# mLSTM attention, soft MoE and a SoLU layer on one core: the first stage in float32 row and column halves, with q and k transposed ahead

## The chip, the cores and the metric

One core of one Trainium2 chip. The time is the device time of one launch in microseconds (us); lower is better. The numbers are the median of three runs and one profiled execution. Engines are named as in the profile: PE (TensorE), PEld (its weight loads), DVE (VectorE), ACT (ScalarE), POOL (GpSimd), SP (SyncE, which issues the DMAs).

## The reference

B = 4 batches, H = 8 heads, S = 768 tokens, head size D = 40, so DM = H x D = 320. Three parts follow one another; the change is in the first.

```python
for t in range(S):                                   # mLSTM, per batch and head
    m_new = max(f_gate[t] + m, i_gate[t])
    f_stab, i_stab = exp(f_gate[t] + m - m_new), exp(i_gate[t] - m_new)
    C = f_stab * C + i_stab * outer(v[t], k[t])
    n = f_stab * n + i_stab * k[t]
    y[t] = sigmoid(o_gate[t]) * (C @ q[t]) / max(abs(n @ q[t]), 1)
x = y.reshape(3072, 320)
logits = x @ phi                                     # soft MoE: 8 experts of 4 slots
d, c = softmax(logits, axis=0), softmax(logits, axis=1)
x = c @ experts(d.T @ x)                             # relu(s @ w1[e]) @ w2[e]
h = x @ w_in                                         # SoLU layer, width 1024
out = layernorm(h * softmax(h), no_mean_shift) * g_ln @ w_out
```

## The kernel before

**Work and tiles.** The tokens are cut into NC = 6 chunks of L = 128. One tile is a chunk of one batch with its 8 heads; the NT = 24 tiles run chunk by chunk, and in a chunk over the B = 4 batches. Inside a tile the recurrence is a matrix product: P = (K Q^T) x W, where W[s, t] is the exponential of gate sums (causal), the numerator is P times values (with a column of ones for the denominator, so HV = 41 columns per head) plus the state of the earlier chunks times q, scaled by a coefficient. Then the state is decayed and k times the decayed values is added.

**Precision.** All matmuls of this stage run in bf16, and every float32 operand is split into a high and a low part. `high` and `low` (L246, L250) read the upper and the lower half of float32 words as bf16. q and k are split and packed to 128 columns per head: Q3 = (qh, qh, ql, 0) and K4 = (kh, kl, kh, kl). ACT writes the high parts (`q_high` L887, `k_high` L897), DVE the low ones (`q_low` L1046, `k_low` L1056). PE transposes both (L612, L613) and ACT copies the result to QKT (L920). So one matmul over 128 rows gives three of the four products of a score (L646), and the state, stacked as C3 by ACT and DVE (L948, L1142), takes q's three parts in one matmul (L654). P is split by DVE (`p_low`, L1075), v by POOL (L455), the decayed values by POOL (L477), x by POOL (L522) and phi once at the start. So P times values is four bf16 matmuls per head (L673 to L676), the update four per head (L690 to L693), x is transposed in six bf16 transposes (L707) and the logits are twelve matmuls (L720).

**Order of the work.** Each engine runs its own list of steps, written by hand: a unit is half a tile (4 heads, UNITS = 8 per chunk), and `step(c, k)` calls the functions of that engine in order, each on the unit that lies its lag behind (`live`, `half`, `tile_of`). The first chunk and the last are written out, the four between are a loop on each engine (`attention_steps`, L254), with addresses from registers. Engines wait for each other by semaphores (`wait_ge`, `then_inc`). DVE's step is at L1202: product of P (L1067), scaling of the state part (L1085), `sum_up` (L1097), low part of P (L1075), |n q| (L1106), q's low part, k's low part, maximum with one (L1115), addition to the state (L1133), reciprocal (L1124), stacked state (L1142). POOL's step decays values (L467) and state (L486), splits them, splits x, gates (L498), splits v and divides (L511). ACT takes the exponentials (L906) and the copies out of PSUM.

**DMAs.** SP loads each tile's q, k and v in one DMA of 484 KB (L337) and one w1 matrix (1280 KB) after each chunk (L363, L364). Behind the stage (`after_attention`) it loads the last two w1, w_out, w2[0] and w_in (L368 to L371), after si_done w2[1] to w2[3] (L374), and after w1_used w2[4] to w2[7] (L377). The expert products L790 (w1) and L822 (w2) are float32 matmuls in four column groups, and for the last 64 rows in two row halves; L802 and L774 are float32 transpositions by matmul with an identity. L822's second half waits for w2[4] to w2[7]. The last stage (from L854) is not touched.

## Time and profile before

| | |
|---|---|
| median of 3 runs | 377.07 us (376.53 to 378.76) |
| profiled execution, its time | 377.63 us |
| its span, first to last instruction | 375.9 us |
| mean granted TensorE clock | 0.909 of 2.4 GHz |
| busy share of the span | PE 74%, PEld 53%, DVE 83%, ACT 64%, POOL 69% |
| DMA | 56.61 MB, mean 151 GB/s |

The span is what the trace covers; the time of the execution is a little more, and the median is that of other runs. A busy share says how long an engine had an instruction in it, not that it set the pace; PE's ends are modelled.

### The profile page before, as it was taken

The page shows a single profiled execution, that of the slowest core. Times are in us where ns is not written, and L with a number is a line of the kernel's source. Part 1 is how long each engine was busy: PE and PEld are TensorE (multiplying, and loading weights), DVE is VectorE, ACT ScalarE, POOL GpSimd, SP SyncE. Part 2 cuts the span into 40 slices and gives each one's busy share as a digit, 9 for nine tenths or more (in the row PEclk, how much of TensorE's full clock was granted, in tenths as well). Part 3 has the DMA queues.
Part 4 walks back from the last instruction along what each step waited for, and adds up shares of the span by engine and source line. Part 5 has one row for each costly group of instructions (what it writes and reads, how often), then busy time and mean ns, then how long its engine had stood idle before and what let it go on. Part 6 is the DMA issues. An engine that isn't in the chain of part 4 may idle for free.

```text
span 375.9 us, 10868 instructions
## 1 busy us (share of the span) xinstructions
PE 279.9 (74%) x3881; PEld 200.6 (53%) x3881; DVE 312.7 (83%) x483; ACT 240.3 (64%) x402; POOL 259.6 (69%) x420
## 2 busy tenths in 40 slices
PE   0048687777878768787787449864838999999996
PEld 0036576666766657576675323421214666666664
DVE  8979999999999999999999654830179999999961
ACT  3857587866678577677766315350158989898970
POOL 4824999988898888889955500941028888888880
PEclk9999988989889698998989859986996999999999
DMA  7901115315113421512450079993009889899994
GB/s 291 365 0 54 56 55 196 107 55 190 55 53 98 157 95 53 192 53 58 138 246 3 2 282 413 418 424 142 0 4 152 175 189 194 181 175 183 201 187 131
DMA packets 62144, 56.61 MB, mean 151 GB/s; under 512 B 52320, under 2 KB 56416, under 8 KB 59552
## 3 DMA queue, kind: packets, MB, share of 16 engines
q1 hardware_dynamic: 62112, 56.19, 51.7%
q8 instruction: 19, 0.31, 0.4%
q14 instruction: 13, 0.11, 0.1%
HBM read 39.66 MB, written 3.93 MB: 116 GB/s over the span
## 4 chain that ended last, share of the span: by engine, by line
DVE 39%; PE 23%; issue 16%; POOL 9%; DMA 7%; ACT 3%; DVEq 1%; SPq 0%; POOLq 0%; ACTq 0%
DVE arena L1056 6%; DMA ring<-w_dram 6%; DVE arena L1142 4%; DVE arena L1106 4%; DVE arena L1115 4%; DVE arena L1067 3%; DVE arena L1075 3%; DVE arena L1097 3%; POOL ring L580 3%; POOL ring L574 3%; PE ps L822 2%; PE ps L863 2%; DVE arena L1133 2%; PE ps L864 2%; PE ps L690 2%
## 5 line engine op out<-in xcount | busy, mean ns | idle before, releaser
L863 PE MATMUL ps<-wouth,ring 128*128 128x320 bf16 x192 | 54.3, 306 | 1.6 <-DMA ring<-ring 1.4
L864 PE MATMUL ps<-woutl,ring 128*128 128x320 bf16 x192 | 54.2, 305 | 0.0
L920 ACT COPY arena<-ps 128x1024 bf16<-128x1024 bf16 x48 | 49.2, 1026 | 5.9 <-PE ps L613 5.6
L612 PE MATMUL ps<-identb,arena 128*128 128x128 bf16 x192 | 30.8, 240 | 24.4 <-DVE arena L1056 24.3
L906 ACT ACTIVATE arena<-ps 128x512 f32<-128x512 f32 x48 | 29.0, 605 | 15.9 <-PE ps L633 15.7
L1075 DVE TENSOR_TENSOR arena<-arena 128x512 bf16<-128x512 f32 x48 | 39.1, 814 | 0.0
L690 PE MATMUL ps<-arena 128*128 128x41 bf16 x160 | 19.2, 187 | 25.8 <-DVE arena L1133 25.8
L1067 DVE TENSOR_TENSOR arena<-ps,arena 128x512 f32<-128x512 f32 x48 | 32.0, 666 | 5.5 <-PE ps L646 3.3
L498 POOL TENSOR_TENSOR arena<-arena,sig 128x320 f32<-128x320 f32 x24 | 27.4, 1142 | 12.5 <-DVE arena L1097 12.3
L1305 DVE TENSOR_REDUCE ring<-ps 128x1 f32<-128x1024 f32 x24 | 29.3, 1223 | 6.1 <-PE ps L854 6.1
L1031 ACT ACTIVATE ring<-ring 128x1024 bf16<-128x1024 f32 x24 | 27.6, 1149 | 10.4 <-POOL ring L593 10.4
L612 PEld LDWEIGHTS ps<-identb,arena 128*128 128x128 bf16 x192 | 20.8, 109 | 24.6 <-issue 24.6
L673 PE MATMUL ps<-arena 128*128 128x41 bf16 x192 | 24.2, 186 | 11.1 <-DVE arena L1075 11.1
L1056 DVE TENSOR_TENSOR arena<-arena 128x640 bf16<-128x640 f32 x24 | 31.2, 1300 | 0.0
L613 PE MATMUL ps<-identb,arena 128*128 128x128 bf16 x192 | 30.7, 239 | 0.0
L690 PEld LDWEIGHTS ps<-arena 128*128 128x128 bf16 x160 | 15.9, 99 | 27.4 <-issue 22.9
L867 PE MATMUL ps<-wouth,ring 128*128 128x320 bf16 x192 | 30.0, 299 | 0.0
L1313 DVE SCALAR_TENSOR_TENSOR ring<-ps,ring 128x1024 f32<-128x1024 f32 x24 | 29.2, 1215 | 0.2
L571 POOL TENSOR_TENSOR ring<-ring 128x512 bf16<-128x512 f32 x24 | 28.3, 1179 | 0.9 <-ACT ring L1027 0.9
L467 POOL TENSOR_TENSOR arena<-arena 128x328 f32<-128x328 f32 x20 | 22.3, 1114 | 9.1 <-ACT arena L911 9.1
L1018 ACT ACTIVATE ring<-ps,ring 128x1024 f32<-128x1024 f32 x24 | 26.3, 1095 | 2.8 <-DVE ring L1305 2.8
L863 PEld LDWEIGHTS ps<-wouth,ring 128*128 128x128 bf16 x192 | 19.1, 100 | 15.8 <-DVE ring L1328 6.4
(206 smaller groups left out, 1126.5 us busy)
## 6 DMA issues: line engine op xcount, KB each, us to landing
ring<-w_dram SPq DMA_DIRECT2D x10, 1280.0 KB, 8.1
arena<-qkv_dram SPq DMA_DIRECT2D x24, 484.0 KB, 3.4
sig<-o_gate_dram SPq DMA_DIRECT2D x3, 1280.0 KB, 9.1
arena<-w_dram SPq DMA_DIRECT2D x3, 1280.0 KB, 8.1
sig<-w_dram SPq DMA_DIRECT2D x3, 1280.0 KB, 15.2
out_dram<-ring SPq DMA_DIRECT2D x24, 160.0 KB, 2.3
arena<-w_out_dram SPq DMA_DIRECT2D x1, 1280.0 KB, 12.6
arena<-w_in_dram SPq DMA_DIRECT2D x1, 1280.0 KB, 14.1
```

The costliest lines, as they stand in the source:

```text
L612: pe.transpose(dst[:, j, :], Q3[b][:, h * QW:h * QW + P], identb[:, :])
L613: last = pe.transpose(dst[:, HALF + j, :], K4[b][:, h * KW:h * KW + P], identb[:, :])
L690: pe.matmul(bX[:, cols], first, high(VD[b % 2][:, cols]), start=True, stop=False)
L863: pe.matmul(o, UHT[i % 4][:, j, :], wouth[:, j, :], start=(j == 0), stop=False)
L864: pe.matmul(o, UHT[i % 4][:, j, :], woutl[:, j, :], start=False, stop=False)
L867: mm = pe.matmul(o, ULT[i % 4][:, j, :], wouth[:, j, :], start=False, stop=(j == FJ - 1))
L920: act.copy(QKT[k % 2], bT[k % 2].bitcast(BF16)).then_inc(s["t_copied"], 1)
L1056: dve.tensor_tensor(k4[:, :, :, 1, :], again(heads(tin[b][:, DM:2 * DM], D), 2, 2), k4[:, :, :, 0, :], ALU.subtract).then_inc(s["k_lo"], 1)
L1067: dve.tensor_tensor(PF[(k - 1) % 2], bS, WT[(k - 1) % 2], ALU.mult).then_inc(s["p_ready"], 1)
L1075: dve.tensor_tensor(low(pf), pf, high(pf), ALU.subtract).then_inc(s["pl_ready"], 1)
L1305: dve.tensor_reduce(nmx[i % 3], h_banks(i), AX.X, ALU.max, negate=True).then_inc(s["mx_ready"], 1)
L1313: dve.scalar_tensor_tensor(out=UT[i % 3], in0=h_banks(i), scalar=1.0, in1=ET[i % 2], op0=ALU.mult, op1=ALU.mult, accum_out=usum[i % 3]).th ...
```

## The change

q and k now come from the host already transposed (`qkT`: for each tile two halves of 4 heads, 40 rows, q's and k's columns), and k and v with its ones by token (`kv1`). The split, packing, transposing and copying of q and k on ACT, DVE and PE go, and so do the stacked state C3, the split of the decayed values, of x and of phi. Scores, queries times state, the update, the transposes of x and the logits are float32 matmuls. Heads 0 to 3 lie on rows 0 to 39 and heads 4 to 7 on rows 64 to 103 of the array; PE takes them in turn (`for r in range(2)` inside `for j`), the scores of the two halves into two PSUM banks. The state is 104 rows by 164 columns, and its update writes its two halves from two column halves. P and v stay split in bf16. A step is a whole tile; all loops are written out. The denominator is one reduction over |n q| and a column of ones. The copy of the logits moves from ACT to DVE, the decay of the values reads W's last column instead of exponentials of its own. `num`, `den`, `rden8` and `scaled` have two buffers, W and P two whole tiles. SP loads a tile in three DMAs and a w1 matrix after every second tile, all eight ahead of `after_attention` (the last two went behind it before).

```diff
--- before.py
+++ after.py
...
-        def attention_steps(eng, step):
-            for k in range(UNITS):
-                step(0, k)
-            with eng.Fori(1, NC - 1) as c:
-                for k in range(UNITS):
-                    step(c, k)
-            for k in range(UNITS):
-                step(NC - 1, k)
-            for k in range(UNITS - 1):
-                step(NC, k)
-
...
+        FLUSH = 5
+
+        def attention_steps(step):
+            for n in range(NT + FLUSH):
+                step(n)
...
+            def load_tile(i):
+                b = i % B
+                for r in range(2):
+                    sp.dma_start(qk[b][r * UPPER:r * UPPER + D, :], qkT[i, r]).then_inc(qk_in[b], 16)
+                sp.dma_start(kv[b], kv1[i]).then_inc(kv_in[b], 16)
...
+            for i in range(B, NT):
+                sp.wait_ge(s["i_done"], i - B + 1)
+                sp.wait_ge(s["o_done"], i - B + 1)
+                sp.wait_ge(s["x_done"], i - B + 1)
+                load_tile(i)
+                if i % 2:
+                    e = (i - B) // 2
+                    if e < RING:
+                        sp.dma_start(ring[:, e, :], w1[e]).then_inc(s["w1_first_in"], 16)
+                    elif e < E:
+                        sp.dma_start(w1_place(e), w1[e]).then_inc(s["w1_late_in"], 16)
 
             after_attention(sp)
-            for e in range(RING, E):
...
+            def decay_values(n):
...
+                pool.wait_ge(s["w_ready"], 2 * i + 2)
                 await_(pool, "x_done", i - 1)
-                vd = VD[b % 2]
-                pool.tensor_tensor(heads(vd, HV), heads(v1, HV), again(kdec[b % 2], 2, HV), ALU.mult) \
+                last_token = heads(WT[i % 2], L)[:, :, L - 1]
+                pool.tensor_tensor(heads(VD[i % 2], HV), heads(values_of(b), HV), again(last_token, 2, HV), ALU.mult) \
                     .then_inc(s["vd_ready"], 1)
...
-            def step(c, k):
-                decay(c, k)
-                decay_state(c, k)
-                decayed_low(c, k)
-                x_low(c, k)
-                gate(c, k)
-                split_v(c, k)
-                divide(c, k)
...
+            def step(n):
+                decay_values(n)
+                decay_state(n)
+                split_v(n)
+                gate(n)
+                divide(n)
...
-                await_(pe, "t_copied", n - 1)
-                dst = bT[parity(k)].bitcast(BF16).rearrange("p (j t) -> p j t", t=P)
+            def exponents(n, hf):
+
+                i = tile_at(n, 0)
+                if i is None:
+                    return
+                c, b = i // B, i % B
+                head = b * H + HALF * hf
+                await_(pe, "w_ready", 2 * i + hf)
+                pe.matmul(bE, identb[:, :], causal[:, :], start=True, stop=False)
+                pe.matmul(bE, A3[0:G3, c * L:(c + 1) * L], pick[:, head:head + HALF, :], start=False, stop=False)
                 for j in range(HALF):
-                    h = HALF * hf + j
-                    pe.transpose(dst[:, j, :], Q3[b][:, h * QW:h * QW + P], identb[:, :])
-                    last = pe.transpose(dst[:, HALF + j, :], K4[b][:, h * KW:h * KW + P], identb[:, :])
-                last.then_inc(s["t_done"], 1)
...
+            def scores(n):
...
+                pe.wait_ge(qk_in[b], 32 * (i // B + 1))
+                await_(pe, "p_ready", 2 * i)
                 for j in range(HALF):
-                    last = pe.matmul(bS[:, j * L:(j + 1) * L], qkt[:, HALF + j, :], qkt[:, j, :],
-                                     start=True, stop=True)
+                    for r in range(2):
+                        last = pe.matmul(bS[r][:, j * L:(j + 1) * L], keys_of(b, r, j), queries_of(b, r, j),
+                                         start=True, stop=True)
                 last.then_inc(s["s_done"], 1)
-                if hf == 0:
-                    await_(pe, "i_scaled", i)
-                await_(pe, "c3_ready", i - B + 1)
+                await_(pe, "i_scaled", i)
+                await_(pe, "state_ready", i - B + 1)
                 for j in range(HALF):
-                    h = HALF * hf + j
-                    last = pe.matmul(bI[:, h * HV:(h + 1) * HV], qkt[:, j, :], C3[b][:, h * HV:(h + 1) * HV],
-                                     start=True, stop=True)
+                    for r in range(2):
+                        last = pe.matmul(bI[r][:, j * HV:(j + 1) * HV], queries_of(b, r, j),
+                                         state[b][r * UPPER:r * UPPER + D, j * HV:(j + 1) * HV],
+                                         start=True, stop=True)
                 last.then_inc(s["i_done"], 1)
 
...
-            def add_to_state(c, k):
...
+            def logits(n):
...
+                for kk in range(NP):
+                    last = pe.matmul(bX[:, 400:400 + SLOTS], XT[i % 2][:, kk, :], phif[:, kk, :],
+                                     start=(kk == 0), stop=(kk == NP - 1))
+                last.then_inc(s["lg_done"], 1)
...
+            def add_to_state(n):
...
+                pe.wait_ge(s["vd_ready"], i + 1)
                 await_(pe, "state_ready", i)
-                for h in range(H):
-                    cols = slice(h * HV, (h + 1) * HV)
-                    first, second = K4[b][:, h * KW:h * KW + P], K4[b][:, h * KW + D:h * KW + D + P]
-                    pe.matmul(bX[:, cols], first, high(VD[b % 2][:, cols]), start=True, stop=False)
-                    pe.matmul(bX[:, cols], first, low(VD[b % 2][:, cols]), start=False, stop=False)
-                    pe.matmul(bX[:, cols], second, high(VD[b % 2][:, cols]), start=False, stop=False)
-                    last = pe.matmul(bX[:, cols], second, low(VD[b % 2][:, cols]), start=False, stop=True)
+                await_(pe, "lg_ready", n - 4)
+                pe.wait_ge(s["coefs_ready"], 3)
+                for j in range(HALF):
+                    for r in range(2):
+                        h = r * HALF + j
+                        last = pe.matmul(bX[r * UPPER:r * UPPER + D, j * HV:(j + 1) * HV], kv[b][:, h * D:(h + 1) * D],
+                                         VD[i % 2][:, h * HV:(h + 1) * HV], start=True, stop=True)
                 last.then_inc(s["x_done"], 1)
 
...
+            def transpose_x(n):
...
+                for kk, r0 in enumerate(PARTS):
+                    last = pe.transpose(bM[:, kk * P:(kk + 1) * P], sig[:, i, r0:r0 + P], identf[:, :])
                 last.then_inc(s["xt_done"], 1)
...
-            def step(c, k):
-                exponents(c, k)
-                transpose_qk(c, k)
-                scores(c, k)
-                if isinstance(c, int) and (c, k) == (0, 1):
+            def step(n):
+                exponents(n, 0)
+                scores(n)
+                exponents(n, 1)
+                if n == 0:
                     coefficients()
-                weigh_values(c, k)
-                add_to_state(c, k)
-                transpose_x(c, k)
-                logits(c, k)
+                weigh_values(n)
+                logits(n)
+                add_to_state(n)
+                transpose_x(n)
...
+            def denominator(n):
                 dve.wait_ge(s["num_ready"], i + 1)
-                nq = heads(num, HV)[:, :, D]
-                dve.scalar_tensor_tensor(out=den, in0=nq, scalar=-1.0, in1=nq, op0=ALU.mult, op1=ALU.max) \
-                    .then_inc(s["abs_ready"], 1)
...
+            def copy_logits(n):
+                dve.wait_ge(s["lg_done"], i + 1)
+                dve.wait_ge(s["x_done"], min(n, NT - B))
+                dve.tensor_copy(lg[:, i, :], bX[:, 400:400 + SLOTS]).then_inc(s["lg_ready"], 1)
...
-            def step(c, k):
-                p_product(c, k)
-                if isinstance(c, int) and (c, k) == (0, 2):
+                for r in range(2):
+                    rows = slice(r * UPPER, (r + 1) * UPPER)
+                    last = dve.tensor_copy(gamma[rows], heads(bX[rows, 0:NT * H], H, NT)[:, :, r * HALF:(r + 1) * HALF])
+                last.then_inc(s["coefs_ready"], 1)
+                dve.wait_ge(s["coefs_ready"], 2)
+                dve.memset(bX, 0.0).then_inc(s["coefs_ready"], 1)
+
+            def step(n):
+                p_product(n, 0)
+                if n == 0:
                     copy_coefficients()
-                scale_inter(c, k)
-                sum_up(c, k)
-                p_low(c, k)
-                absolute(c, k)
-                q_low(c, k)
-                k_low(c, k)
-                at_least_one(c, k)
-                add_state(c, k)
-                invert(c, k)
-                stack_state(c, k)
...
```

PE in the first stage, before: two half-tile steps in the loop (L612, L613: transposes of q and k; L646 scores; L654 queries times state).

```order
L630 MATMUL ps<-causal,identb 128x512
L631 ISA
L631 MATMUL ps<-pick_words,arena 128x512
L633 ISA
L633 MATMUL ps<-arena,pick_words 128x128 x4
L612 MATMUL ps<-identb,arena 128x128
L613 MATMUL ps<-identb,arena 128x128
...
L643 REGISTER_ALU
L646 MATMUL ps<-arena 128x128 x4
L654 MATMUL ps<-arena 128x41 x4
```

PE in the first stage of the changed kernel, from the logits of one step into the next (L602 logits, L619 update, L631 transposes of x, L543 to L546 exponents, L560 scores, L567 queries times state).

```order
L602 MATMUL ps<-phif,arena 128x32 x3
L619 MATMUL ps<-arena 40x41 x8
L631 MATMUL ps<-identf,sig 128x128 x3
L543 MATMUL ps<-causal,identb 128x512
L544 MATMUL ps<-pick_words,arena 128x512
L546 MATMUL ps<-arena,pick_words 128x128 x4
L560 MATMUL ps<-arena 128x128 x8
L567 MATMUL ps<-arena 128x41 x8
L543 MATMUL ps<-causal,identb 128x512
L544 MATMUL ps<-pick_words,arena 128x512
L546 MATMUL ps<-arena,pick_words 128x128 x4
```

The transposes of q and k and the register instructions are gone, the scores of all 8 heads stand together between the two halves of the exponents, and logits, update and transposes are 3, 8 and 3 instructions.

DVE in the first stage, before: one tile is two half-tile steps of the loop (L1056 k's low part, L1142 stacked state, L1106 and L1115 the denominator, L1046 q's low part).

```order
L1067 TENSOR_TENSOR arena<-ps,arena 128x512
L1085 TENSOR_TENSOR arena<-ps,arena 128x328
L1075 TENSOR_TENSOR arena<-arena 128x512
L1056 TENSOR_TENSOR arena<-arena 128x16x40
L1142 SCALAR_TENSOR_TENSOR arena<-arena,lo_rows_c 128x328
...
L1097 TENSOR_TENSOR arena<-arena,ps 128x328
...
L1106 SCALAR_TENSOR_TENSOR arena<-arena 128x8
L1046 TENSOR_TENSOR arena<-arena 128x8x40
L1115 TENSOR_SCALAR arena<-arena 128x8
L1133 TENSOR_TENSOR arena<-arena,ps 128x328
L1124 RECIPROCAL arena<-arena 128x8
```

DVE in a step of the changed kernel (L896 product, L914 scaling, L904 low part, L924 sum, L933 denominator, L951 addition to the state, L960 copy of the logits).

```order
L896 TENSOR_TENSOR arena<-ps,arena 128x512
L914 TENSOR_TENSOR arena<-ps,arena 128x328
L904 TENSOR_TENSOR arena<-arena 128x512
L896 TENSOR_TENSOR arena<-ps,arena 128x512
L924 TENSOR_TENSOR arena<-arena,ps 128x8x41
L904 TENSOR_TENSOR arena<-arena 128x512
L933 TENSOR_REDUCE arena<-arena 128x8
L942 RECIPROCAL arena<-arena 128x8
L951 TENSOR_TENSOR arena<-arena,ps 104x164
L960 COPY lg<-ps 128x32
```

Of the thirteen instructions of a tile ten are left, one of them new here (L960), and the addition to the state has half the elements.

## Rows read from the trace of the kernel before

**Rows 1.** Windows: stretch, its us, busy us (records) by engine, clock, DMA, GB/s.
```profile
60.00:80.00 20.00, 15.86 (x313) 13.69 (x314) 20.00 (x34) 13.44 (x27) 17.96 (x22) 0.83 0.27 90
...
250.00:376.00 126.00, 107.77 (x754) 65.02 (x746) 86.39 (x124) 80.59 (x124) 78.30 (x193) 0.94 0.76 155
```

**Rows 2.** Timeline of DVE: start us, us, engine line op out<-in.
```profile
84.53 0.69 DVE L1067 TENSOR_TENSOR arena<-ps,arena 128x512 f32<-128x512 f32 x1 [0.20 <-issue]
...
92.60 0.63 DVE L1067 TENSOR_TENSOR arena<-ps,arena 128x512 f32<-128x512 f32 x1
```

**Rows 3.** Groups of DVE, 60 to 120 us: busy us, mean ns | idle before.
```profile
L1075 DVE TENSOR_TENSOR arena<-arena 128x512 bf16<-128x512 f32 x15 | 12.7, 847 | 0.0
L1056 DVE TENSOR_TENSOR arena<-arena 128x640 bf16<-128x640 f32 x8 | 10.8, 1344 | 0.0
L1067 DVE TENSOR_TENSOR arena<-ps,arena 128x512 f32<-128x512 f32 x15 | 10.0, 664 | 0.7 <-issue 0.6
L1142 DVE SCALAR_TENSOR_TENSOR arena<-arena,lo_rows_c 128x328 bf16<-128x328 bf16 x7 | 7.2, 1027 | 0.0
L1115 DVE TENSOR_SCALAR arena<-arena 128x8 f32<-128x8 f32 x8 | 5.6, 696 | 0.0
L1106 DVE SCALAR_TENSOR_TENSOR arena<-arena 128x8 f32<-128x8 f32 x7 | 5.4, 770 | 0.0
L1085 DVE TENSOR_TENSOR arena<-ps,arena 128x328 f32<-128x328 f32 x8 | 3.9, 484 | 0.0
```

**Rows 4.** Timeline of PE, first stage, from L690 to L612.
```profile
84.28 0.19 PE L690 MATMUL ps<-arena 128*128 128x41 bf16 x1 [0.74 <-DVE arena L1133]
...
85.41 0.38 PE L630 MATMUL ps<-causal,identb 128*128 128x512 bf16 x1
...
86.06 0.22 PE L612 MATMUL ps<-identb,arena 128*128 128x128 bf16 x1
```

**Rows 5.** Timeline of PE, and groups of PEld (217 to 262 us), behind the first stage.
```profile
237.28 0.60 PE L790 MATMUL ps<-ring,arena 128*8 128x512 f32 x2
...
237.82 0.60 PE L790 MATMUL ps<-ring,arena 64*8 64x512 f32 x2
...
237.86 0.60 PE L790 MATMUL ps<-arena 64*8 64x512 f32 x2
...
238.26 0.60 PE L790 MATMUL ps<-ring,arena 64*8 64x512 f32 x2
...
239.57 1.97 PE L802 MATMUL ps<-identf,pick_words 128*128 128x32 f32 x16 [0.68 <-ACT pick_words L999]
...
L802 PEld LDWEIGHTS ps<-identf,pick_words 128*128 128x128 f32 x16 | 1.9, 191 | 1.6 <-ACT pick_words L999 1.6
...
L774 PEld LDWEIGHTS ps<-sum,arena 128*64 128x64 f32 x4 | 0.2, 134 | 0.0
```

**Rows 6.** Groups of POOL, 60 to 120 us.
```profile
L486 POOL TENSOR_TENSOR arena<-arena 128x328 f32<-128x328 f32 x8 | 10.3, 1285 | 0.0
...
L455 POOL TENSOR_TENSOR arena<-arena 128x328 bf16<-128x328 f32 x8 | 8.5, 1061 | 0.0
...
L498 POOL TENSOR_TENSOR arena<-arena,sig 128x320 f32<-128x320 f32 x7 | 8.2, 1171 | 1.2 <-DVE arena L1097 1.1
...
L511 POOL TENSOR_TENSOR sig<-arena 128x320 f32 x8 | 5.8, 723 | 0.0
```

**Rows 7.** Groups of ACT, 60 to 120 us.
```profile
L906 ACT ACTIVATE arena<-ps 128x512 f32<-128x512 f32 x15 | 9.1, 605 | 5.2 <-PE ps L633 5.2
```

**Rows 8.** Chain that ended last, behind the first stage; timeline row of DVE L1187.
```profile
217.33 0.19 ACT lg L938
...
235.79 23.13 DMA ring<-w_dram
...
259.06 1.23 PE ps L822 x5
...
21.91 0.95 DVE L1187 TENSOR_TENSOR arena<-ring 32x768 bf16<-32x768 f32 x1
```

More of the change, by code:

```diff
@@ L432, in _ @@
             pool.wait_ge(s["im_ready"], 1)
-            for b in range(1, B):
-                pool.memset(C3[b], 0.0)
-            for b in range(B):
-                pool.memset(state[b], 0.0)
             pool.wait_ge(s["ll_ready"], 1)
```

582 lines of the change are left out of this document (202 added, 380 removed).

## The prediction

> **What bounds the kernel now.** The profiled execution takes 377.63 us, 1.7 more than its span of 375.9 and 0.6 more than the median of the runs shown; I reckon in the span and set the difference right at the end. A change of under about 1% (3.8 us) can't be told from none here.
>
> I read the busy time by windows first, since the change touches only the first stage. In a window of it DVE is busy 20.00 of 20.00 us, PE 15.86, POOL 17.96, ACT 13.44 [rows 1]: the first stage is bound by DVE. The DVE timeline gives its rate: the same place of the step, the first product of P in a tile, starts at 84.53 and at 92.60 [rows 2], so a tile takes 8.07 us, and 24 tiles fill the time up to the last copy of logits, which ends at 217.52 (217.33 + 0.19) [rows 8]. The groups of DVE say what a tile pays: two products (L1067) of 0.66, two low parts of P (L1075) of 0.85, k's low part (L1056) 1.34, the stacked state (L1142) 1.03, three of L1085's size at 0.48 and q's low part about the same, and two instructions on eight elements, L1106 and L1115, that take 0.77 and 0.70 [rows 3]. These sum to more than 8.07 because the end of one overlaps the start of the next. Last I read the chain behind the stage: 23.13 us of it is the landing of the last w2 loads, after which L822 starts at 259.06 [rows 8].
>
> **The change part by part.** *DVE.* L1056, q's low part, L1142, L1106 and L1115 go; one small reduction replaces the last two, and a copy of the logits comes over from ACT. What is left per tile: 2 x 0.66, 2 x 0.85, scaling and sum 2 x 0.48, adding to the state 0.24 to 0.48 (half the elements of 0.48), and three small ones, for which I take 0.2 each, the size of the logit copy [rows 3, 8]. Sum 4.8 (5.1 at most).
>
> *POOL.* v's low part 1.06, values times decay 1.1 (as L455), gate 1.17, division 0.72, decay of a state half as long 0.64 (half of L486; 1.29 if length doesn't count): 4.7, at most 5.3 [rows 6]. The low parts of x and of the decayed values, and the dummy instruction, go. *ACT.* Two exponentials of 0.61 [rows 7] and one copy: under 2 us. None of these three reaches what PE needs, next.
>
> *PE.* All bf16 work on q, k, state and logits becomes float32. The trace of before has float32 matmuls behind the stage, and there each is two passes (L802's 8 matmuls are 16 records [rows 5]). These sixteen passes with 128 columns of weights and 32 moving columns take 1.97 us, their weight loads 1.9 where one takes 0.191 [rows 5]: (1.9 - 0.19)/15 = 0.11 us from load to load. The loads, not the 32 columns, set that. Streaming 512 columns takes 0.44 per pass (237.82 to 238.26) [rows 5], so 128 columns take 0.11: a pass of the scores is 0.11 either way. Per tile, then:
> - exponents, twice, unchanged: 85.41 to 86.06, 0.65 each [rows 4]: 1.30.
> - scores: 8 matmuls, 16 passes of 0.11. If the two row halves run side by side 0.89, if one after another 1.78. Rows 5 speak for side by side: L790's 64-row matmuls have eight records (four rows of two) starting between 237.82 and 237.86, and the other eight 0.44 later. One row half (c2) has only four column groups in use, so eight at once means that the two row halves ran together. I take 0.89.
> - queries times state: 16 passes with 128-column loads, 0.89 or 1.78. Here loads weigh, not streams. L774, two column halves of 64, has four loads in 0.20 where one takes 0.134 [rows 5]; one after another, 0.055 apart, they would span 0.30. Loads of different parts of the array overlap. I take 0.89.
> - state update: 8 matmuls with 40 columns of weights in two column halves, like L774: 16 passes, 0.4 to 0.8, I take 0.5.
> - P times values: unchanged, 32 passes. With 12 passes of the logits they fill 84.28 to 85.41 [rows 4], 0.0257 each: 0.82.
> - logits: 6 passes of 0.11, 0.67 (12 of 0.026 before); transposes of x: 3 at 0.11, 0.33 (up to 0.64 if such a transposition streams like two passes).
> - changes between whole array and halves: L790 goes from 128-row to 64-row form between 237.28 and 237.82, 0.54, where a pass takes 0.44 [rows 5]: 0.1 each. There are four per step: 0.4.
>
> Sum 5.8 us at the full clock. The Trainium skill, TensorEngine Tiling (Array Packing), section Key Properties, says that a change of tiling mode drains TensorE. The trace agrees in that there is a gap, of 0.10; a drain of the 0.17 us that the skill's TensorE: Matmul & The Clock Gate gives as the fixed part of a single matmul would, as an estimate, make the step 0.3 and the kernel 6 us longer. It changes no term here.
>
> *Clock.* In the first stage of before the granted clock is 0.83 with PE busy 79%; in the last stage, with PE busy 86%, 0.94 [rows 1]. PE as the bound should look like the latter: 12% of the time at 1.2 GHz, where exponents, scores and P times values take nearly twice as long (about 8.3 us a step). 1/(0.88/5.8 + 0.12/8.3) = 6.0 us. I take 6.0 per tile; PE becomes the bound.
>
> *No ring of waits is longer.* Scores of tile n+1 wait for both products of tile n: from the start of scores n, 0.89 + 0.89 + 0.65 + exponential 0.61 + product 0.66 and four handovers, 3.9 of the 6.0. P times values n-1, logits n-4, update n-1 and transposes n-3 stand between and fill PE. The exponents wait for an exponential that ended 2 us earlier. Behind PE's wait for the update's decayed values (L434 of the changed POOL order) stand only the transposes, and the values are ready a step ahead.
>
> *Ends of the stage.* The rows are ready when L1187 ends, at 22.86 (21.91 + 0.95) [rows 8]; before, q's and k's low parts came next, now the first exponents start at once. The first step has no tile behind it and waits for coefficients, their copies and a memset: 2.4 us over a steady step (in the first step DVE adds four copies and the memset between its two products). After the last step has started: 3.3 for exponents, scores and exponents, 2.4 for exponential, product, sum and low part, 0.8 P times values, 0.5 sum, 1.2 gate, 0.7 division, 0.3 transposes, 0.5 copy, 0.7 logits, 0.2 copy, less what overlaps: 10.6. End: 22.9 + 2.4 + 23 x 6.0 + 10.6 = 173.9 against 217.5, so -43.6.
>
> *DMA.* A tile's load grows from 484 KB in one to about 644 KB in three, and a 1280 KB weight load follows every second one; at 0.38 MB/us (twelve loads of 1280 KB in 41.4 us behind the stage, see below) that is about 3.5 us of a 6 us step on average. A load is issued more than a step before its first reader: I cost it nothing; if it came 1 us late each time, 24 us. Two of twelve weight loads move out of the stretch behind the stage into cover. Twelve took from 217.5 to 258.9 (235.79 + 23.13) [rows 8], 3.45 each: -6.9, less about 0.7 for the queue's gap before si_done: -6.2. What is late next there is L822's first half, which would end near 250 on the old scale, before the new 252.8.
>
> Sum: 375.9 - 43.6 - 6.2 = 326.1 span, 327.8 as time of such an execution, 327 as median.
>
> **The rivals.** *A, partial overlap or waits between tiles*: scores run side by side, but the loads of queries times state take turns (+0.9), step 6.9: 23 x 0.9 = 21 us more, 348. For it: the loads' overlap is seen only on column halves. *B, POOL or DVE bound*: the gaps at changes of form vanish behind loads and the clock stays full; PE 5.3, POOL at 4.7 to 5.3: step 5.3, 311. *C, no change*: row halves take turns for everything: 1.30 + 1.78 + 1.78 + 0.82 + 0.67 + 0.8 + 0.33 + 0.4 = 7.9, 8.0 with clock, 44 + 4 us more than the forecast: 375. Against it the eight records at 237.82. *D, slower*: PE's clock. Weight loads of 0.11 against streams of 0.03 could leave the array counted as idle, and the clock at 1.2 GHz throughout: exponents 2.6, scores 1.7, state 0.9, P times values 1.1, logits 0.7, update 0.6, transposes 0.6, changes of form 0.8: 9.0, 23 x 3.0 and 4 at the ends more: 400. It decides from a step of 8.2 us on. Against it: two thirds of the step are streams or short bf16 passes.
>
> **How the numbers follow.** Forecast 0.55, A 0.20, B 0.13, C 0.07, D (with a late tile load on top of A) 0.05. Faster by over 1%: 0.88; within 1%: 0.07; slower: 0.05. The range reaches into A and B, and holds T from 5.2 to 7.3: 309 to 358.
>
> **What would show it.** Right: PE busy over 90% in the first stage, DVE under 85%; 16 score passes within 1 us, record pairs on the two row halves starting together; 5.8 to 6.2 us from step to step; last logits near 174; L822's second half 6 us closer behind it; ACT under 35% busy. Wrong: score passes 0.11 apart one by one (C), PE idle ahead of scores or updates with POOL or DMA as releaser, a granted clock under 0.8 (D), PE idle with POOL at 100% (B).

## The result and the profile after

The changed kernel takes 331.05 us in the median of four runs (328.48 to 331.48), the kernel before, timed with it, 376.8. The ratio is 0.876, with a 95% interval of 0.871 to 0.882: faster by 12.4%. Forecast were 327.0 us and a range of 309 to 358. The profiled execution takes 331.48 us, its span is 329.3.

Windows of the changed kernel, columns as in [rows 1], which holds the first of these windows of before:

```profile
60.00:80.00 20.00, 19.84 (x339) 17.40 (x342) 19.41 (x37) 6.08 (x11) 11.76 (x18) 1.00 0.77 253
80.00:100.00 20.00, 19.84 (x363) 17.60 (x365) 19.09 (x35) 5.62 (x10) 11.61 (x18) 1.00 0.69 217
```

PE went from 15.86 to 19.84 of 20 us and its granted clock from 0.83 to 1.00. DVE is still at 19.1 to 19.4, so from this view alone nobody could say which of the two sets the pace. ACT fell from 13.44 to 5.6 to 6.1, POOL from 17.96 to 11.7.

The PE timeline of one steady step (in the place of [rows 4]; columns start us, us, engine line op; a matmul row with x16 holds 16 passes, and the merged rows of single bf16 matmuls between 80.32 and 81.14 are left out):

```profile
79.65 0.39 PE L543 MATMUL ps<-causal,identb 128*128 128x512 bf16 x1
...
81.14 0.83 PE L602 MATMUL ps<-phif,arena 128*128 128x32 f32 x6
...
81.90 0.51 PE L619 MATMUL ps<-arena 128*40 128x41 f32 x16
...
82.34 0.55 PE L631 MATMUL ps<-identf,sig 128*128 128x128 f32 x3
...
83.48 1.16 PE L560 MATMUL ps<-arena 40*128 40x128 f32 x16
...
84.47 0.99 PE L567 MATMUL ps<-arena 40*128 40x41 f32 x16
...
85.39 0.39 PE L543 MATMUL ps<-causal,identb 128*128 128x512 bf16 x1
```

From L543 to L543 it is 5.74 us, against 8.07 before [rows 2]. Read start to start, as the durations overlap: exponents 0.67, P times values 0.82, logits 0.76, update 0.44, transposes 0.39, exponents with the change of form 0.75, scores 0.99, queries times state 0.92. (The transposes' 0.39 is the distance from L630 to L543, 88.29 to 88.68, in the run without the low-low product; here the record of L543 is missing.) No row has an idle time in brackets: PE waits for nobody, and for no tile load either.

The start is slower. The scores of the first, second and fourth tile:

```profile
23.64 2.08 PE L560 MATMUL ps<-arena 40*128 40x128 f32 x16
...
33.36 2.08 PE L560 MATMUL ps<-arena 40*128 40x128 f32 x16 [1.72 <-DVE arena L896]
...
49.73 1.16 PE L560 MATMUL ps<-arena 40*128 40x128 f32 x16
```

Sixteen passes take 2.08 us instead of 1.16 in the first three tiles, which is the level of 1.2 GHz. (The record of the granted clock begins with its first change, here at 49.7 us; before that the passes tell the level.) PE was busy 24.3 us of the 27 from 23 to 50 us. The kernel before also began its stage at the half level, but only for 4 us: a 512-column matmul takes 0.63 us at 25.07 and 0.39, as in the steady step, from 29.00 on.

```profile
25.07 0.63 PE L630 MATMUL ps<-causal,identb 128*128 128x512 bf16 x1
...
29.00 0.39 PE L630 MATMUL ps<-causal,identb 128*128 128x512 bf16 x1
```

The end of the stage, PE's timeline and the last copy of logits on DVE:

```profile
172.88 0.88 PE L631 MATMUL ps<-identf,sig 128*128 128x128 f32 x3
174.37 1.46 PE L602 MATMUL ps<-phif,arena 128*128 128x32 f32 x6 [0.61 <-ACT arena L805]
```

```profile
175.87 0.19 DVE L960 COPY lg<-ps 128x32 f32<-128x32 f32 x1 [2.58 <-PE ps L602]
```

The last tiles go through transposes, ACT's copy and logits one after the other (the last pass of P times values starts at 168.31, and four logits follow it, at 168.46, 170.26, 172.06 and 174.37), and the clock is granted at half from 172.6 on. The stage ends at 176.06 (175.87 + 0.19), where it was 217.52 [rows 8].

Behind it, two rows of PE's timeline, the first instruction behind those that si_done stands for, and the start of the second half of the w2 product:

```profile
187.52 0.41 PE L679 MATMUL ps<-arena,onesf 128*128 128x32 f32 x2
...
213.17 1.50 PE L733 MATMUL ps<-ring,arena 128*8 128x320 f32 x12 [4.49 <-DMA ring<-w_dram]
```

L733 is the old L822; its second half still waits for the w2 loads, 37.1 us behind the stage's end, where it was 41.5 (217.52 to 259.06) [rows 8].

### The profile page after: what moved, and what is told of

The parts are those of the page before. It is cut to its first block and busy times, and to the rows that moved or that the text cites. A ratio compares the mean times of both kernels' runs of the same rounds, so it can differ in the third digit from the quotient of the medians.

```text
span 329.3 us, 8741 instructions
## 1 busy us (share of the span) xinstructions
PE 276.9 (84%) x3311; PEld 202.9 (62%) x3345; DVE 256.8 (78%) x419; ACT 144.4 (44%) x222; POOL 174.3 (53%) x334
## 5 line engine op out<-in xcount | busy, mean ns | idle before, releaser
L904 DVE TENSOR_TENSOR arena<-arena 128x512 bf16<-128x512 f32 x48 | 64.9, 1351 | 0.0
L896 DVE TENSOR_TENSOR arena<-ps,arena 128x512 f32<-128x512 f32 x48 | 32.9, 686 | 10.9 <-ACT arena L797 8.2
L434 POOL TENSOR_TENSOR arena<-arena 128x328 f32<-128x328 f32 x20 | 15.0, 751 | 45.9 <-ACT arena L797 45.9
L560 PE MATMUL ps<-arena 40*128 40x128 f32 x384 | 30.6, 304 | 1.7 <-DVE arena L896 1.7
L543 PE MATMUL ps<-causal,identb 128*128 128x512 bf16 x25 | 10.6, 424 | 22.3 <-DVE arena L1006 22.3
L805 ACT COPY arena<-ps 128x384 f32<-128x384 f32 x24 | 11.5, 478 | 40.6 <-PE ps L631 40.6
L774 PEld LDWEIGHTS ps<-wouth,ring 128*128 128x128 bf16 x192 | 19.1, 100 | 15.6 <-DVE ring L1148 6.4
L560 PEld LDWEIGHTS ps<-arena 40*128 40x128 f32 x384 | 25.8, 204 | 4.6 <-issue 2.5
L466 POOL TENSOR_TENSOR sig<-arena 128x320 f32<-128x320 f32 x24 | 17.3, 722 | 20.1 <-DVE arena L942 19.7
L456 POOL TENSOR_TENSOR arena<-arena,sig 128x320 f32<-128x320 f32 x24 | 20.8, 865 | 10.7 <-DVE arena L924 10.7
L567 PE MATMUL ps<-arena 40*128 40x41 f32 x384 | 26.1, 285 | 0.0
L567 PEld LDWEIGHTS ps<-arena 40*128 40x128 f32 x384 | 26.0, 206 | 0.0
L875 ACT CAST ring<-ring 128x1024 bf16<-128x1024 f32 x24 | 24.8, 1033 | 0.2 <-DVE ring L1133 0.2
```

Of the source, the lines that this page charges most:

```text
L560: last = pe.matmul(bS[r][:, j * L:(j + 1) * L], keys_of(b, r, j), queries_of(b, r, j), start=True, stop=True)
L567: last = pe.matmul(bI[r][:, j * HV:(j + 1) * HV], queries_of(b, r, j), state[b][r * UPPER:r * UPPER + D, j * HV:(j + 1) * HV], start=True, ...
L774: pe.matmul(o, UHT[i % 4][:, j, :], wouth[:, j, :], start=(j == 0), stop=False)
L896: dve.tensor_tensor(PF[i % 2][:, cols], bS[hf], WT[i % 2][:, cols], ALU.mult).then_inc(s["p_ready"], 1)
L904: dve.tensor_tensor(low(pf), pf, high(pf), ALU.subtract).then_inc(s["pl_ready"], 1)
```

## The experiments

The times are medians of four executions; the kernel before stood at 376.8 to 378.8 us beside them. The profiled execution also gives the stage's end, which is the better measure of an edit of the stage: what lies between it and the end of the span came out near 153 us in some executions and near 155.5 in others, with the same instructions (153.2 in the changed kernel, 155.1, 156.0 and 155.5 in three of the runs below), as the clock was granted at half for more or less of it (a mean of 0.93 in the changed kernel's 153.2 us, 0.87 in the 155.1 and the 156.0, 0.89 in the 155.5).

**1. Is the start's loss the clock?** Warm-up:

```diff
+            pe.wait_ge(s["ll_ready"], 1)
+            for _ in range(30):
+                pe.matmul(bM, identb[:, :], causal[:, :], start=True, stop=True)
             pe.wait_ge(s["rows_ready"], 1)
```

> Thirty 512-column bf16 matmuls into an unused PSUM bank before the first exponents, started when LL is ready (about 13.7 us), so that PE's clock is at 2.4 GHz when the stage begins. Theory (the steps S0 to S3 of the changed kernel were 9.7, 8.2 and 8.2 us apart because the clock was at 1.2 GHz until 49.7 us): steps 1 to 3 fall to 5.7 to 7, last logits 5 to 7 us earlier, time 324 to 326 against 331. Rival (the first steps are slow because they wait for coefficients, loads and copies): under 2 us gained, 329 to 331. A second rival: the idle stretches of the first steps bring the clock down again, then the time stays at 331 too, but the records show short passes in the first scores only.

Measured: 327.51 us (327.05 to 328.75), 3.5 less. The first tiles' scores on PE, and a window:

```profile
22.94 1.16 PE L560 MATMUL ps<-arena 40*128 40x128 f32 x16
...
30.11 1.26 PE L560 MATMUL ps<-arena 40*128 40x128 f32 x16 [2.35 <-DVE arena L899]
```

```profile
31.00:38.00 7.00, 7.00 (x88) 5.49 (x86) 4.83 (x6) 1.00 (x2) 2.62 (x4) 0.51 0.09 25
```

The first step falls from 9.7 to 7.2 us and the stage ends at 169.79, 6.3 earlier. The three steps from the first to the fourth scores take 19.4 us (22.94 to 42.34) where the changed kernel takes 26.1. There is more to gain: the second scores stand 2.35 us idle for DVE's second product, and from 31.0 us on the clock is at half again for 7 us. Part of the median's gain is given back behind the stage (155.1 for 153.2). The kernels without warm-up differ too: in runs 6 and 8 below the clock rose near 40 us instead of 49.7, and the stage of run 6 ended 3.0 us earlier (173.06) at the same 5.74 us a step. Beside that execution the warm-up is worth 3.3 us of stage, not 6.3.

**2. Do the row halves overlap, and is it the order of issue that makes them?** Scores and queries times state, with the half as the outer loop:

```diff
-                for j in range(HALF):
-                    for r in range(2):
+                for r in range(2):
+                    for j in range(HALF):
                         last = pe.matmul(bS[r][:, j * L:(j + 1) * L], keys_of(b, r, j), queries_of(b, r, j),
...
-                for j in range(HALF):
-                    for r in range(2):
+                for r in range(2):
+                    for j in range(HALF):
                         last = pe.matmul(bI[r][:, j * HV:(j + 1) * HV], queries_of(b, r, j),
```

> Scores and queries times state with the row half as the outer loop and the head as the inner one: same 8 + 8 matmuls, same cost each, but four in a row on one row half. Theory (the overlap of the two halves comes from alternating them): scores go from 0.99 to about 1.8 us, queries times state from 0.92 to 1.8, the step from 5.74 to 7.4, time 331 + 23 x 1.7 = 369. Rival (the engine reorders enough to overlap anyway, or the halves never overlapped and a pass costs less than thought): 331 to 334.

Measured: 432.8 us, and 414 to 448 over its four executions: even the fastest is slower than the kernel before. The windows:

```profile
50.00:60.00 10.00, 10.00 (x169) 8.98 (x167) 9.72 (x18) 2.44 (x5) 5.58 (x9) 1.00 0.76 256
80.00:100.00 20.00, 20.00 (x171) 16.98 (x169) 8.55 (x18) 3.31 (x6) 4.06 (x6) 0.50 0.40 132
```

PE is busy all the time in both, but from 64.8 to 293.5 us, the rest of the stage (which ends at 282.97) and 10.5 us behind it, the clock is granted at half, and a step takes 11.41 us. While it was still full, scores and queries times state took 2.60 us (49.47 to 52.07), against 0.99 + 0.92 = 1.91 in alternating order, and a step was at most 6.42 (55.20 to 61.62). So the order itself costs 0.7 us a step, some 16 us; the other 85 are the clock. Thirty-two passes fully one after the other would take about 3.6 (32 x 0.11, an estimate). In this order the halves still overlap in part, where one half's last passes meet the other half's first. The rows show it where scores on rows 64 to 103 (L560) run beside states on rows 0 to 39 (L567):

```profile
50.58 0.30 PE L567 MATMUL ps<-arena 40*128 40x41 f32 x1
50.68 0.27 PE L560 MATMUL ps<-arena 40*128 40x128 f32 x1
50.71 0.28 PE L567 MATMUL ps<-arena 40*128 40x41 f32 x1
```

**3 and 4. Each group alone.** The scores' loops swapped, then those of queries times state.

> The row halves of the scores alone are issued one after the other (four heads of rows 0 to 39, then four of rows 64 to 103); queries times state keep the alternating order. With both in turn the two groups took 2.60 us at the full clock (49.47 to 52.07) in place of 1.91, so some overlap was left. Theory, the loads hide behind the streams less here, because a 128-column stream is as long as its load: +0.4 to +0.7 us per step at the full clock, +10 to +17 us, 341 to 348. Theory on the clock: it fell in the run with both in turn because the order leaves the array half used; then this half of the edit brings part of that, 360 to 400. Rival: the clock falls only with both, and the time stays under 350.

> The row halves of queries times state alone are issued one after the other; the scores keep the alternating order. Theory, here weight loads set the pace and those of one half follow each other, so less is hidden: +0.3 to +0.9 us per step at the full clock, +7 to +20 us, 338 to 351. If the clock falls as it did with both in turn, 360 to 400; rival: it costs nothing (under 333), and the scores' order was the whole of it.

Measured: 346.4 us (single executions 341.0, 343.7, 349.1 and 349.4; the trace is of the first) and 342.7 (342.35 to 343.12), both inside their ranges. The PE timelines, first of the scores in turn, then of the states in turn:

```profile
91.47 1.37 PE L560 MATMUL ps<-arena 40*128 40x128 f32 x13
...
93.94 0.39 PE L543 MATMUL ps<-causal,identb 128*128 128x512 bf16 x1
```

```profile
91.17 1.16 PE L560 MATMUL ps<-arena 40*128 40x128 f32 x16
...
93.55 0.39 PE L543 MATMUL ps<-causal,identb 128*128 128x512 bf16 x1
```

The pair takes 2.47 and 2.38 us in place of 1.91, the steps are 6.28 and 6.20, and the clock stays full in the stage in both. The rival held: the clock falls only with both.

**5. Is it the clock, and can more work bring it back?** Both groups in turn as in 2, and the product with the causal mask issued three times per half:

```diff
+                for _ in range(2):
+                    pe.matmul(bE, identb[:, :], causal[:, :], start=True, stop=True)
                 pe.matmul(bE, identb[:, :], causal[:, :], start=True, stop=False)
```

> Both groups with their row halves in turn, as in the run of 432.8 us, and in each half of the exponents the 128x512 product with the causal mask issued three times instead of once (the first two are overwritten): 4 more streams of 0.22 us, 0.89 us more work per step. Theory, the loss of that run was the clock: too much of its step were passes in which only a row half of the array moves data; with 0.89 us of full streams more in each step the clock stays at 2.4 GHz, the step is 6.42 + 0.89 = 7.3 us, and the time is 331 + 24 x (7.3 - 5.74) = 368 us: more work, 60 us less time. Rival, the fall was chance or comes from the step's length or the idle of other engines: the clock falls again, the step is above 12 us, and the time over 440.

Measured: 369.5 us (367.5 to 369.8), 63 us less than in 2 with 0.89 us more work per step. Its window and one step:

```profile
80.00:100.00 20.00, 20.00 (x279) 16.48 (x278) 15.51 (x28) 4.67 (x9) 8.61 (x13) 1.00 0.62 197
```

```profile
81.30 1.37 PE L562 MATMUL ps<-arena 40*128 40x128 f32 x13
...
83.90 0.61 PE L544 MATMUL ps<-causal,identb 128*128 128x512 bf16 x2
...
88.58 0.60 PE L562 MATMUL ps<-arena 40*128 40x128 f32 x3
```

Scores and states take the same 2.60 us (81.30 to 83.90), the step is 7.28, the clock full. So it was neither the length of that stretch nor that of the step; the full streams are all that was added, and they kept the clock up. What the chip measures there these runs don't say.

**6. Who sets the pace, PE or DVE?** First POOL kept away from DVE's second low part:

```diff
             def split_v(n):
...
                 b = i % B
+                if i > 0:
+                    pool.wait_ge(s["pl_ready"], 2 * i)
```

> POOL waits for both low parts of P of a tile before it splits v of the next. Theory (the second low part of P takes 2.26 us instead of 0.76 because it can't run beside POOL's row of four instructions; PE sets the pace, so it costs nothing): L904 falls to 0.76 us both times, DVE's busy share in the first stage from 95% to 70%, step still 5.74, time 330 to 332. Rival (DVE, busy 5.5 of 5.74 us, sets the pace as much as PE): the step falls by 0.1 or more, 325 to 329. A second rival for the mechanism (PE's reads of P slow DVE's write): L904 stays at 2.26.

Measured: 331.1 us (329.6 to 331.3), no change, and the step is 5.74 as before. DVE's and POOL's timelines in the changed kernel, and then DVE and POOL in this one:

```profile
80.19 0.76 DVE L904 TENSOR_TENSOR arena<-arena 128x512 bf16<-128x512 f32 x1
...
81.20 0.74 POOL L434 TENSOR_TENSOR arena<-arena 128x328 f32<-128x328 f32 x1 [1.36 <-ACT arena L797]
...
81.90 0.46 POOL L446 TENSOR_TENSOR arena<-arena 104x164 f32<-104x164 f32 x1
...
82.16 2.26 DVE L904 TENSOR_TENSOR arena<-arena 128x512 bf16<-128x512 f32 x1
82.32 0.73 POOL L423 TENSOR_TENSOR arena<-arena 128x328 bf16<-128x328 f32 x1
...
83.01 0.81 POOL L456 TENSOR_TENSOR arena<-arena,sig 128x320 f32<-128x320 f32 x1
```

```profile
84.05 0.80 DVE L906 TENSOR_TENSOR arena<-arena 128x512 bf16<-128x512 f32 x1
...
84.93 0.73 POOL L425 TENSOR_TENSOR arena<-arena 128x328 bf16<-128x328 f32 x1 [0.69 <-DVE arena L906]
```

The same instruction takes 0.76 us with POOL idle and 2.26 beside POOL's row L446, L423, L456, and ends at 84.42, 0.60 behind the row's end (83.82). With POOL behind it, it takes 0.80, and DVE's busy time falls from 19.1 to 14.6 of 20. So 1.5 us of DVE's 5.5 per step were a stall, not work; PE sets the pace.

**7. The same from PE's side.** The scores issued twice:

```diff
-                for j in range(HALF):
+                for j in [j for _ in range(2) for j in range(HALF)]:
```

> The 16 score passes of each tile are issued twice (same operands, same banks), nothing else is changed. Theory, PE sets the pace of the stage: the step grows by what the scores take there, 0.92 to 1.0 us, from 5.74 to 6.7, all 24 tiles of it: +22 to +24 us, about 354 us, with DVE's busy share in the stage falling from 19.2 of 20 to about 17. Rival, DVE (5.5 us of instructions per 5.74 us step) sets it as much as PE: PE has only 0.1 to 0.3 us to spare in that case too, so the step would be 6.4 or less and the time 346 or less. A second rival is the clock: with more passes of 40 rows in a step it could fall to 1.2 GHz inside the stage, as it did with the halves in turn; then over 365.

```profile
82.52 2.06 PE L560 MATMUL ps<-arena 40*128 40x128 f32 x32
...
89.15 1.05 PE L560 MATMUL ps<-arena 40*128 40x128 f32 x14
```

Measured: 354.6 us (351.2 to 358.8) for the 354 expected. The step is 6.63 (82.52 to 89.15): sixteen more passes cost 0.89, 0.056 each, half of the 0.11 of one whole-array pass. That is the overlap of the row halves, measured by itself.

**8. One matmul of four taken from P times values.** The product of the two low parts is left out, so the sum lacks that part:

```diff
                     pe.matmul(bO[:, cols], ph, vl, start=False, stop=False)
-                    pe.matmul(bO[:, cols], pl, vh, start=False, stop=False)
-                    last = pe.matmul(bO[:, cols], pl, vl, start=False, stop=True)
+                    last = pe.matmul(bO[:, cols], pl, vh, start=False, stop=True)
```

> P times values without the product of the two low parts: 24 bf16 passes of 41 columns per tile in place of 32 (the kernel leaves out that part of the sum). Theory, PE sets the pace: 8 x 0.0257 = 0.2 us less per step, 5.54, -4.9 us over the stage, about 326 us. DVE's instructions sum to 5.54 there, so DVE should be at 20 of 20 us busy and this is the last gain that PE alone can give. Rival, the step is held by DVE's second low part (2.26 us beside POOL's row): no gain, 330 to 331.

```profile
80.00:100.00 20.00, 20.00 (x344) 17.31 (x341) 19.88 (x37) 5.67 (x11) 12.25 (x19) 1.00 0.76 257
```

Measured: 327.0 us (326.0 to 329.0), the step 5.54 (83.89 to 89.43), both as expected, with DVE at 19.88 of 20. The step followed PE in full even so. Whether it would follow a further cut without POOL's wait of 6 no run shows.

**9. Where do the w1 loads belong?** The last two moved behind the stage again:

```diff
-                    elif e < E:
-                        sp.dma_start(w1_place(e), w1[e]).then_inc(s["w1_late_in"], 16)
...
             after_attention(sp)
+            for e in range(RING, E):
+                sp.dma_start(w1_place(e), w1[e]).then_inc(s["w1_late_in"], 16)
```

> The last two w1 matrices are loaded behind the first stage again, ahead of w_out. Theory (they were worth what the transfers take, 4.4 us in the comparison of the two traces): 335 to 337 against 331; L733's second half starts 41 us instead of 37 us after the last logits. Rival (another chain, by w_out, sets the start there): 331 to 332.

```profile
214.08 6.34 PE L733 MATMUL ps<-ring,arena 128*8 128x320 f32 x64 [5.50 <-DMA ring<-w_dram]
```

Measured: 333.1 us (332.6 to 338.3), 2.1 more, less than the range. The trace, whose span is 1.1 us longer (330.4), says why not 4: its stage ended 3.0 us earlier (173.04), with the clock at full by the third scores, and the second half of the w2 product starts 41.0 us behind it, for 37.1 in the changed kernel. The move is worth 3.9 us.

**10. Fill at the second tile.** On top of 1, sixteen 328-column matmuls into P times values' bank ahead of the second scores:

```diff
+                for _ in range(16 if n == 1 else 0):
+                    pe.matmul(bO[:, 0:H * HV], identb[:, :], causal[:, 0:H * HV], start=True, stop=True)
                 await_(pe, "p_ready", 2 * i)
```

> 30 extra matmuls ahead of the first exponents, as before, and 16 more of 328 columns where PE waits for DVE's first product, ahead of the second tile's scores. Theory, the low clock from 31.0 to 37.9 us came from that wait (27.6 to 30.1 us) and its cost is what is left of the start's loss: the clock stays at 2.4 GHz from 17 us on, the step from second to third scores falls from 7.4 to about 5.8, and the kernel takes 1.5 us less than with the first 30 alone: 325.5 to 326.5 us. Rival, the waits of the second and third step for the chain exponential, product, low part hold them at 7 us whatever the clock: 327 to 328.

Measured: 325.1 us (321.9 to 327.6), but not for the reason given:

```profile
29.86 4.24 PE L558 MATMUL ps<-causal,identb 128*128 128x328 bf16 x16
```

The clock fell at 26.8 us, ahead of the fill, which then took 4.24 us at the half level and put the second scores off from 30.11 to 34.03. The stage ends at 170.46, 0.7 later than in 1; the lower time is the stretch behind it (153.0 for 155.1). The idea failed, and so did its reason: here the clock fell before PE's wait for the product, so that wait isn't shown to be what brings it down in 1. Between 1 and 10 the medians decide nothing.

**11 and 12. All together.** Warm-up, POOL's wait and the three products, once with the fill, and once without it but with DVE's second product of the first tile ahead of the copies of the coefficients (both leave out the product of the low parts, as 8):

```diff
                 p_product(n, 0)
                 if n == 0:
+                    p_product(n, 1)
                     copy_coefficients()
                 scale_inter(n)
                 p_low(n, 0)
-                p_product(n, 1)
+                if n != 0:
+                    p_product(n, 1)
```

> The extra matmuls of the run with warm-up and fill, POOL's wait for the second low part of P before it splits v, and P times values without the product of the low parts (left out of the sum). Theory: PE's step 5.54 with DVE at 4.3 us of instructions and out of the way, so the gains add: -5 (start) and -4.9 (0.2 x 24) from 331: 321 us, the fastest of all. Rival, POOL's row, now started behind DVE's low part, becomes the one that DVE and PE wait for: step 5.7, 325 to 326.

> The 30 extra matmuls ahead of the first exponents, POOL's wait before it splits v, P times values without the product of the low parts (left out of the sum), no fill at the second tile, and in the first tile DVE's second product of P ahead of the copies of the coefficients. Theory: the second tile's scores waited for that product (2.35 us idle in the run with warm-up alone, third start of exponents done by 27.6), which now ends near 27.5 in place of 30.0; so the second scores start near 27.7 and the whole stage moves 2 to 2.5 us forward; with the fill's own cost gone (0.7) as well, 318.5 us against 321.4 of the run that had the fill. Rival: the second step is held by the coefficients (scaling, then decay and state), no gain, 320.5 to 322.

Measured: 321.4 us (318.5 to 323.1) and 321.6 (318.45 to 323.6): ratios to the kernel before of 0.849 (0.842 to 0.855) and 0.852 (0.847 to 0.857), 9.5 us below the changed kernel. The start of the second, on PE:

```profile
28.30 1.16 PE L562 MATMUL ps<-arena 40*128 40x128 f32 x16
...
30.01 1.09 PE L569 MATMUL ps<-arena 40*128 40x41 f32 x16 [0.56 <-DVE arena L918]
```

The second scores start 4.5 us behind the first (23.78) and 1.8 earlier than in 1, the clock is full from 19.6 to 156 us, and the stage ends at 160.81 against 164.93 in run 11. The medians don't show those 4 us, and the two traces aren't of like executions: that of 12 is of its fastest (318.45), that of 11 of its second slowest (322.54), in which the clock was at half from 26.5 to about 33 us. So the theory of run 12 holds in one trace only. The step is 5.53 in both, as in 8: the gains of 1 and 8 add, and POOL's wait, which takes DVE to 15.0 of 20 us, adds nothing to them.

## Why the prediction was right, step by step

**PE sets the pace**: right, shown from both sides (POOL's wait changes DVE by 4.5 us of 20 and the time by nothing; 0.89 us more on PE is 0.89 us of step, and 0.2 less is 0.2). **The PE terms**: forecast 5.8 at the full clock, measured 5.74, just below the 5.8 to 6.2 named as the sign. Scores 0.89 against 0.99, states 0.89 against 0.92, P times values 0.82 both, logits 0.67 against 0.76, update 0.5 against 0.44, transposes 0.33 against 0.39, exponents 1.30 against 1.42. The measured figures hold the changes of form, for which the forecast had 0.4 apart. The overlap of the row halves, read off [rows 5], held. Issued in turn the two groups cost 0.7 more, not the 1.8 of rival C, as they overlap in part even so; an order without any overlap was not run. (C's own sum is off by 2 us: with 8.0 a step it is 23 x 2.0 = 46 above the forecast, not 44.)

**Clock**: one of the two terms that were mis-sized most. From PE's busy share I took 0.94 and 6.0 us a step; it was 1.00 and 5.74, 23 x 0.26 = 6.0 us too many, of which the clock is 4.6 (6.0 for 5.8) and the passes 1.4 (5.8 for 5.74). The last stage, from which I took it, has another mix of work. Rival B had this half right, the full clock, but neither POOL nor DVE bound the step. As for rival D, its mechanism exists: run 2 shows the clock at half from 64.8 us to the stage's end with PE busy 20 of 20 us, and a kernel slower than the one before. What kept it off here is the alternating order (runs 2 to 5); my argument against it, that two thirds of the step are streams, could not tell how near it was.

**The stage's ends**, two misses to the other side. The first scores came at 23.64 as forecast (22.9 + 0.65). From there to the last ones I had 2.4 + 138.0 = 140.4, and it was 139.0 (162.68 - 23.64): -6.0 by the shorter step, -1.8 for three steps without update or logits (5.06 and twice 5.18), and +6.5 at the start, where three steps took 26.1 instead of 3 x 5.74 + 2.4. I had let the stage begin at the full clock; it had not done so before either (half until about 28.4 us), and here it stayed at half until 49.7. Run 1 puts the miss down to that: with the clock up at the start the three steps take 19.4, for the 19.6 reckoned. Why the clock rose so much later than before isn't shown. The wait for the second product, which stands behind the coefficients' copies on DVE, is inside the 2.4; in run 12, without that wait and with no low clock among them, the three steps take 14.3 (23.78 to 38.08). The copies came late as well. ACT's timeline of the changed kernel:

```profile
21.04 2.34 ACT L819 ACTIVATE sig<-sig 128x2560 f32<-128x2560 f32 x1 [3.96 <-DMA sig<-o_gate_dram]
...
24.68 0.84 ACT L824 ACTIVATE ring<-ring 32x768 f32<-32x768 f32 x1
```

and the same two of before:

```profile
16.32 2.34 ACT L966 ACTIVATE sig<-sig 128x2560 f32<-128x2560 f32 x1 [0.92 <-DMA sig<-o_gate_dram]
...
19.97 0.84 ACT L976 ACTIVATE ring<-ring 32x768 f32<-32x768 f32 x1
```

The last third of the output gates lands 4.7 us later, and the coefficients' exponentials and the first exponential of the stage stand behind it. That the larger tile loads ahead of it are the reason is argued, not shown. The end of the stage took 13.4 us from the last scores (162.68 to 176.06) where 9.95 were reckoned: +3.4. The 10.6 of the forecast has one pass through transposes, copy and logits, but four logits follow the last P times values, 1.8 us apart and at the end, at half a clock, 2.3; and it is the plain sum of its terms, from which nothing was taken off for overlap.

**DMA**: -6.2 forecast, -4.4 measured. Ten loads took 37.1 us, and twelve (run 9) 41.0, 3.42 each, as in before. But ten times 3.42 is 34.2: 2.9 us are lost, for which I had 0.7. The windows of the changed kernel and of run 9 around si_done show 1.3 us of it in the next to last column (2.5 us at a DMA share of 0.50):

```profile
187.50:190.00 2.50, 1.42 (x18) 1.13 (x18) 1.05 (x5) 0.42 (x1) 0.00 (x0) 1.00 0.50 123
```

```profile
185.00:188.00 3.00, 1.92 (x18) 0.96 (x21) 1.74 (x5) 0.37 (x2) 0.00 (x0) 0.86 1.02 427
```

With the w1 loads gone the three loads that need nothing land before PE's chain reaches si_done, which the other seven wait for: a new wait in the old one's place. Where the other 1.6 us went isn't shown; 3.42 is an average that holds the queue's start and end too.

**DVE and POOL**: 4.8 us forecast for DVE, 5.5 measured, and a busy share of 96% where I wrote under 85%. Nine of ten terms are right within 0.1 (products 0.69, first low part 0.76, 0.49 and 0.48, the others 0.15 to 0.28); the second low part is 2.26 for 0.85. POOL took less than forecast (L456 0.81 for 1.17, L423 0.73 for 1.06). The figures of before held waits: the same L467 took 0.73 us at 85.31 and 1.22 at 109.60. That they were waits for DVE is argued. The stall cost nothing here, and nothing in run 8 either, with 0.2 us less on PE.

The sum: 326.1 span forecast; stage +2.2 (0.1 - 1.4 + 3.4), loads +1.8, the stretch behind them 116.1 for 116.8, -0.7: 329.4, and 329.3 was measured. The errors were larger than the sum shows: 7.8 us too many in the steps, 11.8 too few at the ends and in the loads.

## What to carry to other kernels

Issue row halves alternately: a pass then costs 0.056 us here, against 0.081 (2.60 / 32) with the halves in turn, and in this kernel the order also kept PE's clock up. When an engine is busy 96% of the time, look for one instruction that is long only in one place before calling it the bound, and test by moving its neighbour. Price a stage's first and last steps on their own, at the clock that PE has there, and ask of every load taken out of a stretch which semaphore the rest of the queue then waits for.

## What was not expected of the hardware

**The clock can stay at half with PE busy all the time**, 216 of the 218 us from its fall to the stage's end (run 2), and comes back when 0.89 us of whole-array streams of 512 columns are added to each step (run 5). The Trainium skill, TensorE: Matmul & The Clock Gate, Part 1, says that the gate follows how busy PE has recently been. Of the profile's busy time that isn't true here: PE was busy 20 of 20 us in both runs, at either level.

**A DVE instruction waited for a whole row of POOL's.** 0.76 us alone, 2.26 beside three POOL instructions that followed each other without a gap, ended 0.60 after the last. The Trainium skill, SBUF — State Buffer, section Who interferes with whom, has the conflict: a DVE instruction with two inputs in SBUF and a POOL instruction that reads SBUF exclude each other, and whoever issues first holds the ports for the whole instruction. The trace agrees in kind, but the wait was for the row and not for the one instruction that was under way at 82.16 (L446, to 82.36).
